# GpSimd makes the low parts and scalings of the rational stage

## What is computed

```python
# batch 8, heads 8, seq 576, head_dim 64, pack 32
def sm_attn(qq, kk, vv):
    s = scale * np.matmul(qq, kk.transpose(0, 1, 3, 2))
    s = s - np.max(s, axis=-1, keepdims=True)
    a = np.exp(s)
    a = a / (np.sum(a, axis=-1, keepdims=True) + 1e-09)
    return np.matmul(a, vv)
p_packed = sm_attn(p, k, v)
out = sm_attn(q, p_packed, p_packed)
x = np.ascontiguousarray(out.transpose(0, 2, 1, 3)).reshape(B * S, H * D)   # 4608 x 512

# rational stage: w_in 512 x 2048, w_out 2048 x 512
h = x @ w_in
P = a[0] + a[1] * h + a[2] * h2 + a[3] * h3
Q = 1.0 + np.abs(b[0]) * np.abs(h) + np.abs(b[1]) * h2
g = P / (Q + 1e-06)
y = g @ w_out

# SoLU stage: w_in 512 x 1024, w_out 1024 x 512
h = y @ w_in
solu = h * softmax(h)
ln = (solu - mu) / np.sqrt(var + 1e-06) * g_ln
result = ln @ w_out
```

## Time and profile before

| | us |
|---|---|
| median of 3 runs | 1309.89 |
| lowest, highest | 1306.91, 1313.9 |
| profiled execution, its own time | 1308.52 |
| its span, first to last instruction | 1306.2 |
| TensorE busy in the span | 1223.0 (94%) |
| VectorE busy | 994.0 (76%) |
| ScalarE busy | 875.5 (67%) |
| GpSimd busy | 306.6 (23%) |

### The profile page before, as it was taken

The page is one execution under the profiler, slowest core; times in us unless marked ns, Lnnn a source line. Parts: engine busy times, 40 slices in busy tenths (PEclk is TensorE's granted clock), DMA queues, the critical chain, the costliest instruction groups (busy, mean ns, idle before and its releaser), DMA issues.

```text
span 1306.2 us, 27621 instructions
## 1 busy us (share of the span) xinstructions
PE 1223.0 (94%) x10944; PEld 1093.4 (84%) x10944; DVE 994.0 (76%) x1670; ACT 875.5 (67%) x1406; POOL 306.6 (23%) x205
## 2 busy tenths in 40 slices
PE   6888776799999999999999999999999999999999
PEld 4556554799999999999999999998888888888887
DVE  4666655899999999999999999976555555555553
ACT  3466555789899898999999999964343434343433
POOL 1333321233333233233333323321111011101100
PEclk8799987799999999999999999999999999999999
DMA  7789963320121211212112121102111111111100
GB/s 272 244 309 307 323 224 106 141 67 29 57 77 45 67 43 44 77 44 68 51 35 77 44 92 36 43 10 66 34 48 48 44 36 48 48 44 36 48 33 33
DMA packets 68254, 114.27 MB, mean 87 GB/s; under 512 B 7728, under 2 KB 38448, under 8 KB 68144
## 3 DMA queue, kind: packets, MB, share of 16 engines
q1 hardware_dynamic: 68144, 112.75, 26.1%
HBM read 72.36 MB, written 40.37 MB: 86 GB/s over the span
## 4 chain that ended last, share of the span: by engine, by line
PE 48%; DVE 27%; issue 13%; ACT 11%; DMA 1%; POOL 0%; SPq 0%; ACTq 0%; DVEq 0%
DVE num L1008 6%; DVE rec L1005 6%; PE ps_h L72 6%; PE ps_h L74 6%; PE ps_h L73 6%; PE ps_o L72 5%; PE ps_o L74 5%; PE ps_o L73 5%; DVE den L997 4%; ACT rec L917 3%; DVE num L992 3%; PE ps_s L353 3%; ACT rec L920 3%; PE ps_s L366 3%; PE ps_t L1250 2%
## 5 line engine op out<-in xcount | busy, mean ns | idle before, releaser
L72 PE MATMUL ps_y<-g_hi,wout_hi 128*128 128x288 f32 x1024 | 306.3, 299 | 16.7 <-ACT y_out L949 16.7
L959 POOL TENSOR_TENSOR den<-den,h_abs 128x576 f32<-128x576 f32 x128 | 202.9, 1585 | 450.8 <-ACT den L912 450.8
L73 PE MATMUL ps_y<-g_lo,wout_hi 128*128 128x288 f32 x1024 | 304.3, 297 | 0.0
L74 PE MATMUL ps_y<-g_hi,wout_lo 128*128 128x288 f32 x1024 | 303.6, 296 | 0.0
L72 PEld LDWEIGHTS ps_y<-g_hi,wout_hi 128*128 128x128 f32 x1024 | 194.3, 190 | 19.9 <-issue 19.8
L74 PEld LDWEIGHTS ps_y<-g_hi,wout_lo 128*128 128x128 f32 x1024 | 195.0, 190 | 0.0
L73 PEld LDWEIGHTS ps_y<-g_lo,wout_hi 128*128 128x128 f32 x1024 | 194.5, 190 | 0.0
L72 PE MATMUL ps_h<-x_hi,wp_hi 128*128 128x288 f32 x512 | 154.8, 302 | 5.7 <-DVE wp_lo L974 5.7
L73 PE MATMUL ps_h<-x_lo,wp_hi 128*128 128x288 f32 x512 | 153.1, 299 | 0.0
L74 PE MATMUL ps_h<-x_hi,wp_lo 128*128 128x288 f32 x512 | 152.3, 298 | 0.0
L912 ACT ACTIVATE den<-h_abs,kept 128x576 f32<-128x576 f32 x128 | 111.4, 871 | 38.4 <-DVE rec L1005 38.2
(11 more groups left out here) (121 smaller groups left out, 2612.4 us busy)
## 6 DMA issues: line engine op xcount, KB each, us to landing
wp_scratch<-wp_out SPq DMA_DIRECT2D x32, 512.0 KB, 5.6
wp_lo<-wp_scratch SPq DMA_DIRECT2D x32, 512.0 KB, 4.0
k_main<-in_k SPq DMA_DIRECT2D x16, 576.0 KB, 6.7
q_main<-in_q SPq DMA_DIRECT2D x16, 576.0 KB, 5.6
v_main<-in_v SPq DMA_DIRECT2D x16, 576.0 KB, 5.1
y_scratch<-y_out SPq DMA_DIRECT2D x16, 576.0 KB, 3.4
y_lo<-y_scratch SPq DMA_DIRECT2D x36, 256.0 KB, 3.0
out<-result SPq DMA_DIRECT2D x36, 256.0 KB, 2.1
```

What stands on the lines that cost most here:

```text
L72: pe.matmul(out, lh, rh, start=first, stop=False)
L73: pe.matmul(out, lh, rl, start=False, stop=False)
L74: return pe.matmul(out, ll, rh, start=False, stop=last)
L959: pool.tensor_tensor(den[s % 2][:, :, :], den[s % 2][:, :, :], h_abs[s % 2][:, :, :], ALU.mult)\
```

## The change

All low parts of W' and x from step 0 on, the scaling of weight slices and their low parts go from VectorE's queue to GpSimd's, each behind the `den` product of the same step. Only the first split of x and of W' block 0, before step 0, stay on VectorE. The arithmetic is the same, instruction by instruction. ScalarE's, TensorE's and SyncE's queues are not touched.

```diff
-    def gpsimd(pool, last_steps):
+    def splits_gpsimd(pool, s):
+        for bt, n, k in splits_at(s):
+            split_block_lo(pool, bt, n, k)
+        if x_split_at(s) is not None:
+            split_x_lo(pool, x_split_at(s))
+
+    def gpsimd(pool, slices, last_steps):
         for s in range(EARLY, STEPS):
             step_gpsimd(pool, s)
+            splits_gpsimd(pool, s)
+            slices(pool, s)
             last_steps(pool, s)
...
-    def extras_vector(dve, s, slice_lo):
-        for bt, n, k in splits_at(s):
-            split_block_lo(dve, bt, n, k)
-        if x_split_at(s) is not None:
-            split_x_lo(dve, x_split_at(s))
-        slice_lo(dve, s)
-
-    def vector(dve, slice_lo):
+    def vector(dve):
         for s in range(EARLY, STEPS + LAG):
             step_vector(dve, s)
-            extras_vector(dve, s, slice_lo)
...
-    def early_vector(dve, s):
-        step_vector(dve, s)
-        for bt, n, k in splits_at(s):
-            split_block_lo(dve, bt, n, k)
+    def early_gpsimd(pool, s):
+        step_gpsimd(pool, s)
+        splits_gpsimd(pool, s)
...
-    def slices_vector(dve, s):
+    def slices_gpsimd(pool, s):
...
             for h in range(2):
                 half = stage[:, h * DM:(h + 1) * DM]
-                mm = dve.tensor_scalar(half, half, gain_in[:, 2 * n + h:2 * n + h + 1], None, ALU.mult)
+                mm = pool.tensor_scalar(half, half, gain_in[:, 2 * n + h:2 * n + h + 1], None, ALU.mult)
...
-            dve.wait_ge(slice_hi_ready, n + 1)
-            dve.tensor_tensor(lo, stage, hi.bitcast(F32), ALU.subtract).then_inc(slice_lo_ready, 1)
+            pool.wait_ge(slice_hi_ready, n + 1)
+            pool.tensor_tensor(lo, stage, hi.bitcast(F32), ALU.subtract).then_inc(slice_lo_ready, 1)
```

More of the change, by code:

```diff
@@ L960, in step_gpsimd, with split_x_lo, split_block_lo @@
             .then_inc(den_ready, 1)
-    def gpsimd(pool, last_steps):
+    def splits_gpsimd(pool, s):
[4 more added lines that the diff above has]
+    def gpsimd(pool, slices, last_steps):
         for s in range(EARLY, STEPS):
             step_gpsimd(pool, s)
+            splits_gpsimd(pool, s)
+            slices(pool, s)
             last_steps(pool, s)
-    def split_x_lo(dve, q):
-        dve.wait_ge(x_hi_ready, q + 1)
-        dve.tensor_tensor(x_lo[q % 2][:, :, :], x_raw(q), x_hi[q % 2][:, :, :].bitcast(F32), ALU.subtract)\
+    def split_x_lo(eng, q):
+        eng.wait_ge(x_hi_ready, q + 1)
+        eng.tensor_tensor(x_lo[q % 2][:, :, :], x_raw(q), x_hi[q % 2][:, :, :].bitcast(F32), ALU.subtract)\
             .then_inc(x_lo_ready, 1)
-    def split_block_lo(dve, bt, n, k):
-        dve.wait_ge(block_hi_ready, 2 * BLOCKS * bt + 2 * n + k + 1)
-        dve.tensor_tensor(wp_lo[n][:, k, :], block_raw(n)[:, k, :], wp_hi[n][:, k, :].bitcast(F32), ALU.subtract)\
+    def split_block_lo(eng, bt, n, k):
+        eng.wait_ge(block_hi_ready, 2 * BLOCKS * bt + 2 * n + k + 1)
+        eng.tensor_tensor(wp_lo[n][:, k, :], block_raw(n)[:, k, :], wp_hi[n][:, k, :].bitcast(F32), ALU.subtract)\
             .then_inc(block_lo_ready, 1)
@@ L1034, in rational_block @@
                 first_hi=first_hi, first_lo=first_lo, negate=negate, magnitudes=magnitudes, biases=biases,
-                early_scalar=early_scalar, early_vector=early_vector, early_gpsimd=step_gpsimd, store_y=store_y,
+                early_scalar=early_scalar, early_vector=step_vector, early_gpsimd=early_gpsimd, store_y=store_y,
                 y_to_sbuf_act=y_to_sbuf_act, ring_at=ring_at, vec_at=vec_at,
@@ L1172, in slices_vector @@
             if n == 0:
-                dve.wait_ge(gain_loaded, 16)
-            dve.wait_ge(slice_in, 16 * (n + 1))
+                pool.wait_ge(gain_loaded, 16)
+            pool.wait_ge(slice_in, 16 * (n + 1))
             for h in range(2):
                 half = stage[:, h * DM:(h + 1) * DM]
-                mm = dve.tensor_scalar(half, half, gain_in[:, 2 * n + h:2 * n + h + 1], None, ALU.mult)
+                mm = pool.tensor_scalar(half, half, gain_in[:, 2 * n + h:2 * n + h + 1], None, ALU.mult)
             mm.then_inc(slice_scaled, 1)
@@ L1376, in solu_norm_block @@
                 guard=guard, gain_to_sbuf=gain_to_sbuf, first_h=first_h, slice_load=slice_load,
-                first_tiles=first_tiles, slices_vector=slices_vector, slices_scalar=slices_scalar,
+                first_tiles=first_tiles, slices_gpsimd=slices_gpsimd, slices_scalar=slices_scalar,
                 first_splits_gpsimd=first_splits_gpsimd)
@@ L1423, in _ @@
             attention["gpsimd"](pool, rational["early_gpsimd"])
-            rational["gpsimd"](pool, solu_norm["first_splits_gpsimd"])
+            rational["gpsimd"](pool, solu_norm["slices_gpsimd"], solu_norm["first_splits_gpsimd"])
             solu_norm["gpsimd"](pool)
@@ L1429, in _ @@
             attention["vector"](dve, rational["negate"], rational["first_lo"], rational["early_vector"])
-            rational["vector"](dve, solu_norm["slices_vector"])
+            rational["vector"](dve)
             solu_norm["vector"](dve)
```

## The result

| | before | after |
|---|---|---|
| median, us | 1311.49 (4 runs) | 1375.01 (4 runs) |
| lowest to highest | 1306.91 to 1313.9 | 1372.88 to 1377.44 |
| profiled execution, its own time | 1308.52 | 1372.88 |
| its span | 1306.2 | 1371.1 |
| first \|h\| (line 906) of step 0 starts | 200.61 | 204.02 |

The changed kernel takes 1.0489 times the time of before, with a 95% interval of 1.0453 to 1.0525. The forecast of 1371 and its range of 1346 to 1393 hold it.

The account below looks back on a forecast made before the run. TensorE and VectorE both seemed the bound, with a 4.57 us loop over ScalarE and VectorE setting plain steps. 1308.5 of the profiled execution + 54.7 (stage) + 7 (start) = 1370, forecast as 1371, range 1346 to 1393.

Parts of the forecast that it names:

- The mechanism: Rational stage: GpSimd's low part, reading SBUF, holds VectorE up in line 1005 by 1.10 us, inside the loop.
- The stage: Rational stage, 123 intervals between line 1008 starts: 618.2 us now, 672.9 after, 54.7 more.
- the term of a step with W': Rational stage, 49 steps with a low part of W' alone: 5.67 us each, 277.8 together.
- Scaling steps: Rational stage, 4 steps with two scalings: 1.0 us per scaling, both in the loop, 6.5 a step, 26.0 together.
- The boundary in step 3 of a batch, and x behind it: Rational stage: 6.0 us for a step with low part and two y copies, 4.57 plain, 5.79 with x.
- The boundary in step 11: Rational stage: a step with low part and two y copies at 6.0 us, then one with W' at 5.67.
- Slice low parts: Rational stage, 8 steps: line 1008 waits about 2.2 us, 6.5 a step (ends 5.67 and 7.0), 52.0 together.
- The start: First steps: block 1's second low part queues on GpSimd, TensorE resumes 4.8 us later; 7 us in all (3 to 9).
- No stall: Rational stage: low parts don't hold VectorE, steps 4.80 us by TensorE, its 16.7 of waits go; about 1300; 5%.
- The clock: TensorE's lower clock after 15 chunk boundaries delays `h` by 1 to 2.5 us each, 15 to 37 more; 1386 to 1408; 15%.
- The hold beside the loop: Rational stage: GpSimd holds line 1008 instead of 1005, steps 5.5 us, 57 steps save 0.2 to 0.4; 1348 to 1360; 15%.
- The loop of 4.48: Plain step before: ScalarE's `den` to VectorE's line 1005 and back, 4.48 us plus 0.09 for hand-overs; other products lie outside.

Follow-up runs that it names:

- The memset: Changed kernel, with GpSimd's low parts of W' from step 5 on replaced by a memset that writes and reads nothing: 1317.99 us, ratio 1.0056.
- the four single parts: Kernel before, moving to GpSimd only W' from step 4 (1357.61 us), only x (1319.68), only slices (1313.18), or only W' in steps 0, 1, 3 (1314.29).
- x alone: Kernel before, with only the 15 low parts of x moved to GpSimd: 1319.68 us, ratio 1.0068.
- the kernel with W' alone: Kernel before, with only the low parts of W' from step 4 on moved to GpSimd: 1357.61 us, ratio 1.0365.
- the kernel with the earlier copy of y: Kernel before, with ScalarE's first copy of y at a chunk boundary ahead of that step's logarithm and exponential: 1309.47 us, ratio 0.9989.
- the kernel with the wait for `rec`: Changed kernel, with GpSimd's low parts of W' (from step 5 on) and x waiting until line 1013 of that step is done: 1364.69 us, ratio 1.0434.

## Why the prediction was right, and where only its sum was

**The mechanism held.** The forecast stood on one row of before, line 1005 at 1.85 us beside line 1272, and on the timing by which GpSimd's low part would come there every time. Both were there: 5.67 us a step in 42 steps (the sum had 49; the first of each batch is longer), line 1013 up to 1.86 with W' and 1.99 with x. (The prediction took the 0.62 behind GpSimd's end for the product's own length, which is 0.75; the sum didn't use it.) Line 1013 is longer than 1.2 us 60 times, line 1016 23 times. The memset shows that GpSimd's reading instruction is needed for it, and the four single parts that nothing else is hidden in the total. The Trainium skill (SBUF — State Buffer, "Who interferes with whom") says that a VectorE instruction with two SBUF inputs contends with a GpSimd instruction that reads SBUF and not with one that only writes; the 1.85 beside the low part and the 0.75 beside the memset agree.

**The stage:** 672.9 predicted, 673.2 measured. That it is so close is luck: the term of a step with W' was right, and others were off by up to 6 us and cancelled.
- *Scaling steps.* Predicted were 6.5 and then a plain 4.57; measured 5.00 and 4.79, so 5.1 us too much over four times. What failed is "let both stand in the loop". The two scalings hardly hold VectorE:

```profile
267.15 3.97 POOL L1176 TENSOR_SCALAR y_out<-y_out,kept 128x512 f32<-128x512 f32 x2
267.86 1.16 DVE L1009 TENSOR_TENSOR g_lo<-num,g_hi 128x576 fp32r<-128x576 f32 x1
268.94 0.75 DVE L1013 SCALAR_TENSOR_TENSOR rec<-den,rec 128x576 f32<-128x576 f32 x1
269.72 1.13 DVE L1016 SCALAR_TENSOR_TENSOR num<-num,kept,rec 128x576 f32<-128x576 f32 x1
...
273.73 3.01 POOL L1182 TENSOR_TENSOR wout_lo<-y_out,wout_hi 128x1024 fp32r<-128x1024 f32 x1 [1.21 <-ACT wout_hi L1191]
274.51 2.85 DVE L1016 SCALAR_TENSOR_TENSOR num<-num,kept,rec 128x576 f32<-128x576 f32 x1
```

  Each holds VectorE by 0.3 to 0.4, together 0.7, but takes 1.85 to 2.14 us of GpSimd, outside the bounds of 0.48 to 1.29 that the prediction gave. The 1.0 that was taken for each was too small for GpSimd and too large for VectorE, and the estimate of 769 ns that the prediction set beside it was further off for GpSimd.
- *The boundary in step 3 of a batch, and x behind it.* For the three steps there the sum had 6.0 + 4.57 + 5.79 = 16.36. They take 5.0, then 5.3 to 6.5, then mostly 6.36, together 6.2 us more over seven batches. Two things are in it. One is the lower clock, 4.4 us. The other is the step with x, 6.36 where x alone makes 5.81; the 0.55 between is there without x too, in the kernel with W' alone (5.12 instead of 4.57), and isn't there in the kernel with the memset, where x is 5.81 again. ScalarE waits 0.80 to 0.87 us for TensorE's h just before. So "TensorE's waits grow, and cost nothing by themselves: it is a step and more ahead" didn't hold behind waits of 4.5 us. How much of the 0.55 is the clock and how much the wait stays open.
- *The boundary in step 11.* 6.0 + 5.67 = 11.67 predicted, 5.0 + 6.55 measured (once 7.56): right as a sum, placed otherwise. In both kinds the hold fell on line 1016, for 1.72 and 1.87 us, as predicted.
- *One step with x too many.* The sum has eight. GpSimd makes the first in step 5, ahead of the line 1016 with which the stage begins: 1.2 us too much.
- *Slice low parts.* 6.5 predicted, 6.42 measured, with the hold on line 1016 as predicted (2.85 us, last row above). GpSimd takes 3.01 there and 2.80 for the other four, instead of the 2.39 of the earlier trace rows.
- *The rest.* Plain steps and the last boundary are 0.8 us over the sum.

**The start:** 7 predicted (3 to 9), 6.4 measured, 5.6 alone. In the changed kernel the wait of 5.70 has become 10.35 at 223.44, 4.65 more, where 4.8 was predicted.

**The rivals.**
- *No stall.* `rec` wasn't at 0.75. The kernel with the memset shows most of that case: the stage is 616.1, and without the 6.1 and 2.1 that x and the slices cost alone it would be 607.9, an estimate, 10 us under before and not 16.7. With the start's 5.6 to 6.4 that leaves some 4 us under before, about 1305 from the 1308.5 of the profiled execution. The rival's 1300 took all of TensorE's waits for gain; the kernel with the earlier copy of y shows that they aren't.
- *The clock.* It came in part. Behind six of the 15 boundaries a step is 0.7 to 1.2 us longer where the granted clock is 0.53 to 0.66 over the 7 us in front, 5.4 us together; the rival wanted 1 to 2.5 behind each of the 15, and 15 to 37 us.
- *The hold beside the loop.* The kernel with the wait for `rec` makes that case, and gives 1364.7, not 1348 to 1360. The rival's step of 5.5 was right (5.53). It expected 0.2 to 0.4 from each of 57 steps and more from the scalings. A step with W' gained 0.14, and the scalings lost: with the low part behind them and one of x they take 6.08 + 7.85 + 4.58 = 18.5 us, where the changed kernel takes 16.2 without that x. The stage is 9.9 us shorter in all. The loop of 4.48 in the prediction told rightly which row ends last, but as a bound it was incomplete: VectorE's own load stands 0.2 us behind it.

## What to carry to other kernels

VectorE lost by an instruction that it no longer had to make, though GpSimd was idle most of the time. So an engine's idle share is no free room where its work can hold another engine up: look in the trace for one place where the pair already overlaps, read the length of the held instruction there, and count that for every instruction that you move. If the engine that is held is nearly full, it matters little where the hold falls, and the move that paid here is to make the instruction vanish into one that is run anyway (the scale of an activation), not to hand it on. Before you move a term into another queue, write down what stands ahead of it there at the one place where someone waits for it.

## What was not expected of the hardware

- A GpSimd memset of 128x512 (0.53 us) beside two-input products of VectorE leaves them at 0.75 us; a two-input product of GpSimd of the same size makes one 1.85.
- GpSimd's scaling of 128x512, with one input, took 1.85 to 2.14 us beside a busy VectorE, longer than its two-input product of that size (mostly 1.44), and held VectorE by only 0.3 to 0.4 each time. VectorE's line 1013 ran through at 0.75 inside it. The Trainium skill (SBUF — State Buffer, "Who interferes with whom") has the second instruction wait for the whole length of the first; these rows don't show that for the scaling. Whether the two took turns, and what GpSimd's extra time is, stays open.
- A two-input product of GpSimd of 128x256 took 1.02 us where one of 128x512 at the same place took 1.44, and the shortest of each were 0.79 and 1.26: halving it saves 0.42 to 0.47, not half.
- TensorE at the lower clock behind a wait of 4.49 us (0.53 over 7 us) made a step 6.46 us long, and 5.29 behind a like wait with a clock of 0.78, although TensorE wasn't the bound of the stage.
- A wait in front of GpSimd's low part, by which it starts 0.05 us after VectorE's product (586.09 against 586.04), still made VectorE's product 1.95 us long.
